# Attention and a routed expert layer in one kernel: the last tile's scores as row tiles in two rounds, transposes by row tiles, the first expert's weights loaded behind a scatter, routing in three-operand forms

## What is computed

```
scores = q @ k^T / sqrt(64)          # 4 x 8 heads, 576 x 576
scores = scores where >= rowmax - tau, else -1e9
x      = softmax(scores) @ v         # -> (2304, 512): 4 batches x 576 tokens
logits = x @ w_gate + bias[modality]; e = argmax(logits)      # 8 experts
y      = softmax(logits)[e] * (relu(x @ w1[e]) @ w2[e])       # F1 = 1024
out    = mish(y @ w_in) @ w_out                               # F2 = 2048
```

## Time and profile before

| | |
|---|---|
| time, median of 3 runs | 951.7 us (951.16 to 951.82) |
| time of the profiled execution | 950.58 us |
| its span, first to last instruction | 948.9 us |
| busy in the span | PE 97%, PE weight loads 81%, DVE 71%, ACT 54%, POOL 50% |
| mean granted TensorE clock | 0.995 |

### The profile page before, as it was taken

The page is one execution under the profiler, slowest core; times in us unless marked ns, Lnnn a source line. Parts: engine busy times, 40 slices in busy tenths (PEclk is TensorE's granted clock), DMA queues, the critical chain, the costliest instruction groups (busy, mean ns, idle before and its releaser), DMA issues.

```text
span 948.9 us, 19389 instructions
## 1 busy us (share of the span) xinstructions
PE 919.1 (97%) x6976; PEld 771.2 (81%) x6977; DVE 675.5 (71%) x1227; ACT 509.0 (54%) x987; POOL 476.6 (50%) x560
## 2 busy tenths in 40 slices
PE   6999998999999999999999989999999999999996
PEld 4777776777778788888878878889898889899985
DVE  7999998999966411111152898878888788788793
ACT  5777777778752422222254564545545455555552
POOL 5222244657332654000000586786777777776884
PEclk9999999999999999999999999999999999999999
DMA  4131346232124573111225100100001000000000
GB/s 130 55 100 51 102 140 239 97 108 85 42 83 169 143 272 92 46 37 47 80 86 218 45 1 1 35 34 19 24 27 35 33 2 0 34 1 1 34 1 34
DMA packets 21937, 65.97 MB, mean 70 GB/s; under 512 B 3552, under 2 KB 3552, under 8 KB 21600
## 3 DMA queue, kind: packets, MB, share of 16 engines
q1 hardware_dynamic: 14512, 39.90, 12.3%
q0 software_dynamic: 4896, 20.00, 6.2%
q10 hardware_dynamic: 2448, 5.01, 1.9%
HBM read 46.63 MB, written 18.27 MB: 68 GB/s over the span
## 4 chain that ended last, share of the span: by engine, by line
PE 61%; DVE 4%; issue 4%; ACT 1%; ACTq 1%; POOL 0%; POOLq 0%; DVEq 0%
PE psum L1417 6%; PE psum L1419 6%; PE psum L1418 6%; PE psum L1409 6%; PE psum L1407 6%; PE psum L1408 6%; PE psum L1080 3%; PE psum L1082 3%; PE psum L1081 3%; PE psum L1107 3%; PE psum L1109 3%; PE psum L1108 3%; DVE rr L1529 2%; PE psum L1091 2%; PE psum L1066 1%
## 5 line engine op out<-in xcount | busy, mean ns | idle before, releaser
L1529 DVE RECIPROCAL rr<-rr 128x384 f32<-128x384 f32 x96 | 244.1, 2543 | 10.0 <-ACT rr L1477 10.0
L1355 POOL TENSOR_TENSOR uu<-uu,ex 128x384 f32<-128x384 f32 x96 | 97.2, 1013 | 100.9 <-ACT uu L1471 100.8
L577 ACT ACTIVATE prob<-ssb,smin 128x576 f32<-128x576 f32 x144 | 111.6, 776 | 66.5 <-DVE ssb L699 66.3
L1407 PE MATMUL psum<-x2T_hi,w_in_hi 128*128 128x384 f32 x384 | 131.0, 341 | 4.3 <-DVE gg L1535 2.7
L1409 PE MATMUL psum<-x2T_hi,w_in_lo 128*128 128x384 f32 x384 | 129.6, 338 | 0.0
L1408 PE MATMUL psum<-x2T_lo,w_in_hi 128*128 128x384 f32 x384 | 129.1, 336 | 0.0
L1161 DVE TENSOR_TENSOR hT_lo<-psum,hT_hi 128x512 fp32r<-128x512 f32 x38 | 26.3, 691 | 140.6 <-ACT hT_hi L1138 135.5
L699 DVE TENSOR_SCALAR_CACHE_REDUCE ssb<-psum,tauk 128x576 f32<-128x576 f32 x144 | 112.1, 812 | 12.7 <-PE psum L422 11.0
L339 POOL TENSOR_TENSOR limit<-smin,margin 128x2 f32<-128x2 f32 (+1 forms) x80 | 57.4, 718 | 120.4 <-DVE ssb L699 119.8
L1417 PE MATMUL psum<-w_hi,g_hi 128*128 128x512 f32 x288 | 114.5, 397 | 0.0
L1477 ACT ACTIVATE rr<-uu 128x384 f32<-128x384 f32 x96 | 50.5, 526 | 118.6 <-POOL uu L1355 118.6
(11 more groups left out here) (210 smaller groups left out, 2126.5 us busy)
## 6 DMA issues: line engine op xcount, KB each, us to landing
qk<-in_qk_dram SPq DMA_DIRECT2D x15, 640.0 KB, 3.9
vsb<-in_v_dram SPq DMA_DIRECT2D x16, 512.0 KB, 3.5
xrow<-xs ACTq DMA_DIRECT2D x17, 288.0 KB, 2.9
ys<-ysb SPq DMA_DIRECT2D x19, 257.0 KB, 3.0
stage<-in_w_in_dram POOLq DMA_DIRECT2D x16, 256.0 KB, 4.0
wa<-in_wa_dram SPq DMA_DIRECT2D x8, 512.0 KB, 7.0
wb<-in_wb_dram SPq DMA_DIRECT2D x8, 512.0 KB, 10.7
xs<-zrow SPq DMA_DIRECT2D x11, 288.0 KB, 2.8
```

The source lines that it names most:

```text
L577: act.activation(prob[:, n % 3, cols], ssb[:, w, cols], ACT.Exp, bias=smin[:, w, h:h + 1], scale=-1.0).then_inc(exp_done, 1)
L1407: pe.matmul(bank_of(n), w_in_hi[:, k, cols], xT_hi[w][:, k], start=(k == 0), stop=False)
L1529: dve.reciprocal(rr[:, n % 4], rr[:, n % 4]).then_inc(r_done, 1)
```

## The change

1. Every tile is transposed by halves. by_half goes, and so do the whole transposes and their copies on ACT.
2. A last tile's scores become four matmuls on row tiles instead of two on the whole array. Each PSUM bank takes both heads' part in one accumulation, so they run in two rounds: round one (begin_rest) writes head 0 into bank 0 and head 1 into bank 1, and round two, the other way round, adds to what is there. Round one is called from within turn, in the middle of the transposes of the tile with n % 5 == 1, and it is there that PE now waits for DVE's copies of the step. Round two stands where the scores stood, and waits for round one.
3. LOAD_AT goes from 40 to 45. SPLIT_AT was steps 46 to 54 and 61 to 67, and is now 50 to 54 and 61 to 71.
4. Ten DVE instructions of each batch's routing, tensor_tensor, tensor_copy and tensor_scalar on 128x40 or 128x5 elements, become scalar_tensor_tensor with a neutral third operand.

```diff
-LOAD_AT = ROUTE + RANK + 8
+LOAD_AT = ROUTE + RANK + 13
-SPLIT_AT = [c for c in range(LOAD_AT + 6, NS) if ...][:2 * PIECES]
+SPLIT_AT = [c for c in range(LOAD_AT + 5, NS) if ...][:2 * PIECES]
...
-            if n >= 2:
+            if n >= 2 and tt < QT:
                 pe.wait_ge(copied, units(n))
...
             else:
+                pe.wait_ge(rest_begun, p + 1)
                 qr = qk[:, u, 2 * S:]
-                pe.matmul(a_bank[:, 0, :], qr, k[:, 0:HALF], start=True, stop=True)
-                pe.matmul(a_bank[:, 1, :], qr, k[:, HALF:S], start=True, stop=True).then_inc(scores_done, 1)
+                pe.matmul(a_bank[:, 1, :], qr[0:D], k[0:D, HALF:S], start=False, stop=True)
+                pe.matmul(a_bank[:, 0, :], qr[D:P], k[D:P, 0:HALF], start=False, stop=True).then_inc(scores_done, 1)
+        def begin_rest(n):
+            u, k = n // TT % 2, k_of(n // TT % 2)
+            pe.wait_ge(copied, units(n))
+            qr = qk[:, u, 2 * S:]
+            pe.matmul(a_bank[:, 0, :], qr[0:D], k[0:D, 0:HALF], start=True, stop=False)
+            pe.matmul(a_bank[:, 1, :], qr[D:P], k[D:P, HALF:S], start=True, stop=False).then_inc(rest_begun, 1)
...
                 for b in range(1, blocks):
                     if b == QT:
                         pe.wait_ge(prob_done, units(n + 1))
+                        if between:
+                            between()
...
-                turn(c - 2)
+                turn(c - 2, (lambda: begin_rest(c + 1)) if (c + 1) % TT == QT else None)
...
-                dve.tensor_tensor(le[:], lg[:], m, ALU.subtract).then_inc(le_done, 1)
+                dve.scalar_tensor_tensor(le[:], lg[:], 0.0, m, ALU.add, ALU.subtract).then_inc(le_done, 1)
...
-                note(dve.tensor_copy(x[:, b % 2, :, ID_COL], ids[:, tts]))
+                note(dve.scalar_tensor_tensor(x[:, b % 2, :, ID_COL], ids[:, tts], 0.0, ids[:, tts], ALU.add, ALU.max))
```

More of the change, by code:

```diff
@@ L51 @@
 SCATTER_AT = RANK + 3
-LOAD_AT = ROUTE + RANK + 8
+LOAD_AT = ROUTE + RANK + 13
 CLEAR_AT = (ROUTE + RANK + 4) // TT + 2
 PIECES = WCOLS // 512
-SPLIT_AT = [c for c in range(LOAD_AT + 6, NS) if not SCATTER_AT <= (c - ROUTE) % PER <= SCATTER_AT + TT][:2 * PIECES]
+SPLIT_AT = [c for c in range(LOAD_AT + 5, NS) if not SCATTER_AT <= (c - ROUTE) % PER <= SCATTER_AT + TT][:2 * PIECES]
 ALL_CONSTS = 18
@@ L183, in attention_phase @@
     far_turned = sem("far_turned")
+    rest_begun = sem("rest_begun")
     main_out = sem("main_out")
@@ L221, in turned_block @@
     def turned_block(n, b):
[L223 to L226, removed]
+        return both_halves(n % 2, b * D, D, FAR)
     rank_bank, moved = psum[:, 7, 0:(TT + 1) * E], psum[:, 7, (TT + 1) * E:(TT + 1) * E + 1]
@@ L437, in turn @@
             blocks = QT if not full else 2 * QT
[L439 to L470, removed]
+            def half_block(place, h, b):
+                rows = slice(h * D, h * D + D)
+                key = b * P if b < QT else (S + REM + (b - QT) * P if b < 2 * QT else QT * P)
+                return pe.transpose(place, prob[rows, w, key:key + P], ident[rows, rows])
@@ new lines, in turn @@
+            if full:
+                half_block(rest_bank[:, D:2 * D], 1, 0).then_inc(far_turned, 1)
+            else:
+                half_block(turn_bank[:, 1, 0:D], 1, 0)
+            half_block(turn_bank[:, 0, 0:D], 0, 0)
+            for b in range(1, blocks):
+                if b == QT:
+                    pe.wait_ge(prob_done, units(n + 1))
+                    if between:
+                        between()
+                at = b - full
+                half_block(turn_bank[:, 1, at * D:at * D + D], 1, b)
+                half_block(turn_bank[:, 0, b * D:b * D + D], 0, b)
@@ L472, in pv @@
+            at = blocks - full
+            half_block(turn_bank[:, 1, at * D:at * D + D], 1, 2 * QT)
+            if full:
+                pe.wait_ge(far_turned, halved(n))
+                half_block(rest_bank[:, 0:D], 0, 2 * QT).then_inc(turned, 1)
+            else:
+                half_block(turn_bank[:, 0, QT * D:QT * D + D], 0, 2 * QT).then_inc(turned, 1)
         def pv(n):
@@ L584, in evacuate @@
                 act.wait_ge(pv_done, n - 1)
[L585 to L588, removed]
+            if n % TT < QT:
                 act.copy(pt[:, w, QT * P:QT * P + P], rest_bank).then_inc(rest_out, 1)
@@ L765, in choose @@
             elif k == 1:
-                step(dve.tensor_tensor(lg[:], lg[:], lg_b[:], ALU.add))
-                note(dve.tensor_tensor(lg[:], lg[:], btok[:, tts, :], ALU.add))
+                step(dve.scalar_tensor_tensor(lg[:], lg[:], 0.0, lg_b[:], ALU.add, ALU.add))
+                note(dve.scalar_tensor_tensor(lg[:], lg[:], 0.0, btok[:, tts, :], ALU.add, ALU.add))
             elif k == 2:
@@ L770, in choose @@
             elif k == 3:
[L771 to L773 removed]
+                dve.scalar_tensor_tensor(le[:], lg[:], 0.0, m, ALU.add, ALU.subtract).then_inc(le_done, 1)
+                step(dve.scalar_tensor_tensor(oh[:, TT:2 * TT], lg[:], 0.0, m, ALU.add, ALU.is_equal))
+                note(dve.scalar_tensor_tensor(oh[:, TT:2 * TT], oh[:, TT:2 * TT], 1.0, er, ALU.mult, ALU.mult))
             elif k == 4:
```

15 lines of the change are left out of this document (7 added, 8 removed).

## The result

| | before | after |
|---|---|---|
| time, median | 951.4 us (4 runs, 950.97 to 951.82) | 960.4 us (4 runs, 959.85 to 960.99) |
| profiled execution, its span | 950.58, 948.9 us | 960.99, 959.3 us |
| PE, DVE, ACT busy | 97%, 71%, 54% | 96%, 71%, 53% |
| mean granted clock | 0.995 | 0.991 |

The ratio is 1.0095 (95% interval 1.0077 to 1.0112), so the change costs 9.0 us. The forecast was 955.0 with a range up to 957.4: the sign was right, the size well short, and the time lies outside the range.

What follows compares the result with a forecast made beforehand. The prediction took each pair to be bound by a loop of DVE's score copies and PE's work after them. Rounds with halves +5.8, load -3.6 and new hold +1.06 gave +3.3 us: 951.7 to 955.0, range 950.4 to 957.4.

Steps and rivals of the forecast that it cites:

- What bounds it: Attention pair: DVE's copy, then PE's work from 47.36 to 55.11 sets the pace; PE's earlier transposes do not.
- Halves at 0.05 per pair: Transposes ahead of DVE's copy: halves save 0.39 us of PE work per pair, only 0.05 credited.
- the rest turns into idle time of PE: Ahead of DVE's copy: beyond the 0.05 credited, PE's saved 0.39 us per pair becomes waiting, given no cost.
- The rounds: Last tile's scores to product with v: 1.59 us instead of 1.12, net 0.42 more per pair.
- How often: Cost per pair: in full in nine pairs, 3.8 us; 0.29 in seven others, 2.0 us; together +5.8.
- The last tile's copy at nothing: Last tile's scores come out 0.4 us later, at about 48.97, their copy starts at 49.17; cost taken as zero.
- The load: Steps 46 to 49: weights issued in step 45 no longer delay scatters; 3.57 us go, no new wait.
- Pieces and forms: Routing: moved POOL pieces add a hold in step 72, +1.06 us; three-operand forms cost zero and stay held.
- PE as the bound: Rival, attention: PE's work counts everywhere, so the kernel gets faster, -7.0 us to 944.7; chance 0.13.
- the unheld forms: Rival, routing: three-operand forms are not held up by POOL, 4.0 us off, 951.0 us; chance 0.12.
- the lower bound of the rounds: Rival, last tile's scores: passes of 0.24 throughout, rounds cost 3.1 us, total +0.6, 952.3 us; chance 0.16.
- the rival with a new wait: Rival: wa late in step 50, or PE's instructions late once; a us or two, 956.5 to 957.5; chance 0.05.

Runs made afterwards that it cites:

- e4: Kernel before with all transposes by halves, the last tile's scores as before; 950.51 us, 0.9993 of the kernel before.
- e5: Changed kernel with round one behind all the transposes of the step instead of among them; 957.51 us, 1.0057 of the kernel before.
- f1: Changed kernel with old scores for the first pair's last tile and no POOL piece beside the ids' instruction; 951.87 us, 1.0017 of the kernel before.
- e11: Kernel before with the load behind the scatter and no POOL piece beside the ids' instruction, without halves; 946.95 us, 0.9950 of the kernel before.
- e1: Kernel before with only the later expert-weight load (LOAD_AT and SPLIT_AT as after); 948.67 us, 0.9971 of the kernel before.
- e2: Kernel before with only the three-operand forms of the routing instructions; 951.69 us, 0.9999 of the kernel before.
- e7: Changed kernel with already done half transposes repeated in PE's idle time of steps 53 and 73, holds kept; 958.57 us, 1.0060 of the kernel before.
- e6: Changed kernel with the POOL pieces of steps 51 and 71 moved away from the ids' instruction; 955.99 us, 1.0024 of the kernel before.
- e9: Changed kernel with the old scores for the last tile of the first pair alone; 957.69 us, 1.0065 of the kernel before.
- f3: Changed kernel with only the piece of step 71 moved, so the hold of step 52 stays; 954.98 us, 1.0046 of the kernel before.
- f4: Changed kernel with only the piece of step 51 moved, so the hold of step 72 stays; 956.66 us, 1.0067 of the kernel before.
- e10: Changed kernel with the last tile's scores on the whole array in one round at their old place; 949.66 us, 0.9983 of the kernel before.
- e8: Kernel before with halves, the load behind the scatter and no POOL piece beside the ids' instruction; 947.54 us, 0.9959 of the kernel before.

## Why the prediction was wrong

- **What bounds it.** Right. DVE's copy ends last, PE idles ahead of L428, and the time from there to the product with v sets the pair.
- **Halves at 0.05 per pair.** The credit was too high (e4: the scores start 0.04 earlier and the product with v at the same 48.48), and harmless. The sentence behind it, "the rest turns into idle time of PE", is where the forecast failed.
- **The rounds.** 1.59 forecast, 1.53 measured; 0.42 per pair forecast, 0.46 measured. The working was not right in its parts: the ten transposes were summed at 0.36 and round one at 0.59, but without the transposes the distance between the rounds stays 0.83 (e5). The reader should take the wait for round one's end as the price, with the transposes hidden behind it. The sum agreed partly by luck.
- **How often.** Too high for the pairs behind routing: 2.0 for seven. f1 against e11 shows 1.07 for six of them, three of these nothing. "The last tile's copy at nothing" was off too: 0.15 of the 0.46 shows there already.
- **The load.** -3.57 forecast, -3.9 measured in e1 and -3.76 in the changed kernel, no wait in its place.
- **Pieces and forms.** +1.06 forecast, +1.08 measured. Forms at zero (e2), and held by POOL as before. The Trainium skill, SBUF — State Buffer, section Who interferes with whom, was weighed there for two SBUF inputs; the trace agrees, 1.23 us for L799 beside L368. The COPY with one input that it replaces took 1.23 as well.
- **The step that failed** is that idle time of PE was priced at nothing. The hold (1.07 of idle time) and PE's new order (0.84, of it 0.43 by the halves and the rest by the early wait) each stay without a drop by themselves. Together they make 2.09 us in steps 53 and 73, beside which the clock fell in 7 of 9 places, and in e7 2.7 us came back when a part of that idle time was filled. By e6 the two places cost 6.1 us where the holds themselves cost 2.1: 4 us that no term had (1.4 and 1.9 of it seen as clock in the profile after, the rest with the stall of step 77, whose cause is open). The early wait in the first pair costs another 1 to 3: 2.2 by e9, 0.7 by f1 against e6, and between tiles 3 and 6 1.9 to 2.8 in five of its seven profiles, 0.5 and 3.3 in the others. The forecast had the clock in its own rows: the window of 0.51 behind the 2.31 us wait. It was read as a loss that goes, not as what other idle time of that size can cost.
- **The sum.** Load -3.9, rounds +4.7, new hold +1.1, clock and stall behind the holds +4.0, first pair +1 to +3: 7 to 9 us, against 8.4 to 9.0 measured. The last two terms come from intervals of 1 to 2 us either way, so the sum closes no better than that. The top of the forecast's range was set a little wide of its own sum: -3.6 + 7.9 + 1.06 above 951.7 is 957.1, not 957.4.

The rivals: PE as the bound is refuted by e4, the unheld forms by e2 and by the 1.23 of L799, the lower bound of the rounds (0.25 per pair) by the 0.46. Of the rival with a new wait, wa was in time in step 50; "the instructions of PE arrive late once" is perhaps the stall of step 77.

**What stays open.** Why the stall of 2 us in step 77 is in the five profiles with rounds and pieces in both steps 51 and 71 (the changed kernel twice, e5, e7, e9) and in none of f3, f4, e6 or e10. The profiles of before, e6, e8, e10 and e11 have a shorter one of 1.0 to 1.2 us between tiles 76 and 78. The trace after shows a DMA packet of instructions at 271.86 between the scatters, but such packets are there in the others too. Why the clock dropped behind 2.09 us in step 73 in all four profiles and in step 53 in three of five, and why not behind 2.24 to 2.26 in the last layer. And what the two rounds would cost if round two did not wait by a semaphore for round one.

## What to carry to other kernels

Idle time of PE is not free: before an edit makes PE wait longer, or earlier, add the new wait to every other delay that can fall on the same step, and compare the sum with the idle times beside which the clock has dropped in your traces. It tells where a drop is possible, not that it comes. Parts that are harmless alone can do harm together, and two parts can remove the same wait, so a test of parts one by one does not give the whole; run the whole with one part taken out as well. Here a group of matmuls split into two rounds, the second waiting for the first, paid for the first round's end, with ten transposes between them or none.

## What was not expected of the hardware

- In steps 53 and 73, idle times of 2.09 us went with a fall to the 1.2 GHz level in 7 of 9 places, 1.68 to 1.69 us in 2 of 5, up to 1.26 us in none of 22. Such a drop cost 1.2 to 1.9 us. In the last layer 2.72 us went with one in 14 of 18, and 2.24 to 2.26 us in none of 4. The Trainium skill, TensorE: Matmul & The Clock Gate, section HAM oscillation — how this bites in real kernels, tells of waits in a loop that put the clock down each time round; these traces agree that a wait can do it, but here it was a single wait of 2.09 us, and not each time.
- More work made the kernel faster: 48 repeated transposes in idle time saved 2.7 us (e7).
- Executions of one kernel on one core differ by up to 6 us. The two profiles of the changed kernel differ by 1.7 us in the first six steps, of the 3.5 between these executions: the last stretch at 1.2 GHz before a long one at full clock ended at 20.2 and 22.9 us in these two, and at 7.0 in the profile before and 13.4 in that of e1.
